# fp32 attention ahead of two MLPs: raw fp32 scores on row tiles, values held stationary on column tiles, GpSimd dividing the probabilities

## What is computed

```
scores = scale * q @ k^T                      # q and k are about 3 in size
scores = where(0 <= i - j < 128, scores + slope[head] * -(i - j), -1e9)
attn   = exp(scores - rowmax);  attn = attn / (rowsum + 1e-9)
x      = (attn @ v), heads side by side       # 2304 x 512
x      = gelu-like MLP (512 -> 2048 -> 512) of x
out    = a second MLP of the same sizes, with another activation
```

## Time and profile before

| what | value |
|---|---|
| median of 3 runs | 852.1 us |
| the profiled execution's own time | 850.05 us |
| its span, first to last instruction | 848.2 us |
| PE busy | 841.0 us (99%), 5744 matmuls |
| DVE, ACT, POOL busy | 711.7 us (84%), 538.4 us (63%), 116.5 us (14%) |
| granted TensorE clock | full in all 40 slices |
| attention | about the first 140 us |

### The profile page before, as it was taken

How to read it: one execution, slowest core, us unless ns; L and a number is a source line. 1 busy time by engine, 2 the same in 40 slices (tenths; PEclk the granted TensorE clock), 3 DMA queues, 4 the chain that set the end, 5 groups by cost and what they waited for, 6 DMA issues and landing times.

```text
span 848.2 us, 15510 instructions
## 1 busy us (share of the span) xinstructions
PE 841.0 (99%) x5744; PEld 836.5 (99%) x5744; DVE 711.7 (84%) x982; ACT 538.4 (63%) x791; POOL 116.5 (14%) x82
## 2 busy tenths in 40 slices
PE   8999999999999999999999999999999999999998
PEld 8999999999999999999999999999999999999998
DVE  7888898786988966778998897989989789889794
ACT  7778787676776546767744556767556566765441
POOL 3788988000000000000000000000000000000000
PEclk9999999999999999999999999999999999999999
DMA  8978671667776347686764862587646643888822
GB/s 199 227 207 227 186 187 68 257 256 283 241 256 223 135 163 273 241 303 246 261 241 185 298 227 122 199 282 267 233 162 247 231 153 141 296 290 295 304 106 75
DMA packets 63257, 186.45 MB, mean 220 GB/s; under 512 B 7504, under 2 KB 14352, under 8 KB 59344
## 3 DMA queue, kind: packets, MB, share of 16 engines
q1 hardware_dynamic: 62896, 185.30, 64.0%
q10 hardware_dynamic: 288, 0.16, 0.1%
HBM read 113.09 MB, written 72.35 MB: 219 GB/s over the span
## 4 chain that ended last, share of the span: by engine, by line
PE 91%; DVE 5%; POOL 1%; issue 1%; ACT 0%; DMA 0%; SPq 0%; DVEq 0%; POOLq 0%
PE ps L1075 79%; PE ps L1043 5%; PE ps L1009 3%; PE ps L1022 3%; DVE arena L1755 1%; POOL qk_hi L895 1%; PE ps L1037 1%; DVE probs L1645 1%; POOL k_lo L892 1%; PE ps L1052 1%; DVE qk_hi L1613 0%; DVE raw_first L1714 0%; DVE g L1787 0%; DMA qk_raw<-qkT 0%; DVE raw_first L1709 0%
## 5 line engine op out<-in xcount | busy, mean ns | idle before, releaser
L1075 PE MATMUL ps<-arena,w_first 128*128 128x384 f32 x1764 | 328.4, 336 | 0.0
L1075 PEld LDWEIGHTS ps<-arena,w_first 128*128 128x128 f32 x1764 | 307.3, 188 | 1.0 <-DVE arena L1755 0.6
L1075 PE MATMUL ps<-arena,w_rest 128*128 128x384 f32 x1260 | 240.0, 336 | 0.1
L1075 PEld LDWEIGHTS ps<-arena,w_rest 128*128 128x128 f32 x1260 | 220.1, 188 | 0.8 <-DVE arena L1755 0.4
L1755 DVE TENSOR_TENSOR arena<-raw_first,arena 128x768 fp32r<-128x768 f32 (+1 forms) x114 | 148.8, 1319 | 74.4 <-ACT arena L1333 74.1
L1333 ACT ACTIVATE arena<-raw_first 128x768 fp32r<-128x768 f32 (+1 forms) x120 | 132.0, 1117 | 46.1 <-DVE raw_first L1714 39.0
L1075 PE MATMUL ps<-w_rest,arena 128*128 128x256 f32 x945 | 130.8, 280 | 0.2 <-DVE g L1858 0.2
L1075 PEld LDWEIGHTS ps<-w_rest,arena 128*128 128x128 f32 x945 | 119.5, 189 | 0.4 <-issue 0.4
L1075 PE MATMUL ps<-w_first,arena 128*128 128x256 f32 x567 | 86.2, 279 | 0.0
L1755 DVE TENSOR_TENSOR arena<-raw_rest,arena 128x1536 fp32r<-128x1536 f32 (+1 forms) x48 | 71.3, 1486 | 7.1 <-ACT arena L1333 7.0
L1333 ACT ACTIVATE arena<-raw_rest 128x1536 fp32r<-128x1536 f32 (+1 forms) x48 | 60.9, 1269 | 22.4 <-PE ps L1075 20.2
(11 more groups left out here) (125 smaller groups left out, 971.0 us busy)
## 6 DMA issues: line engine op xcount, KB each, us to landing
gd<-g SPq DMA_DIRECT2D x24, 1536.0 KB, 6.1
raw_rest<-gd SPq DMA_DIRECT2D x32, 768.0 KB, 5.1
wst<-w_pairs SPq DMA_DIRECT2D x32, 512.0 KB, 5.7
raw_first<-gd SPq DMA_DIRECT2D x16, 768.0 KB, 6.0
yd<-ust SPq DMA_DIRECT2D x6, 1536.0 KB, 6.3
qk_raw<-qkT SPq DMA_DIRECT2D x30, 288.0 KB, 3.9
wd<-ust SPq DMA_DIRECT2D x4, 1536.0 KB, 8.8
raw_first<-yd SPq DMA_DIRECT2D x4, 1536.0 KB, 7.2
```

The costliest lines, as they stand in the source:

```text
L1075: last = nc.tensor.matmul(to, stationary, moving, start=start and n == 0, stop=n == len(steps) - 1, skip_group_check=True)
```

## The change

- Queries and keys are loaded once for both heads of a pair (head 0 on partitions 0 to 63, head 1 on 64 to 127), kept as plain fp32, and neither rounded nor split. Each score tile is one fp32 matmul over 64 rows; the two heads are issued alternately and lie on two row tiles of the array, each with its own PSUM bank.
- `accum_out` of the exponential gives the row sums. DVE adds 1e-9 and inverts them, once for items 0 to 3 and once for 4 to 8 of a pair, and POOL multiplies each of the nine items by its inverse, in place.
- PE transposes the divided probabilities (16 transposes a pair, in groups of four); ACT copies head 0's to `probs_t` and DVE head 1's.
- The values become the stationary operand (128x64) and the transposed probabilities the moving one (256, 128 or 64 columns), fp32, on two column tiles: head 0's output on partitions 0 to 63, head 1's on 64 to 127. The output is then already in the layout of `x_pairs`: the five last transposes go, and one DVE copy of 128x576 remains.
- The order goes by pairs. On PE: scores of pair q in two groups, transposes of q-1 (first group), values of q-2, transposes of q-1 (second group). `dve_gate` is now raised ahead of each of the nine items.
- At the seam the first two P1 products come ahead of the last transposes and values, then P6, P6, P5. The splits of S1 and S2 and the sums around them are placed anew among POOL, ACT and DVE; the split of S2 moves from POOL to DVE.

The core of the diff:

```diff
@@ PE: scores @@
-                for n_pass, k in enumerate((keys(qk_hi, head), k_lo[:, head % SPLIT_RING])):
-                    last = nc.tensor.matmul(place, queries, k[:, key0:key0 + BAND],
-                                            start=n_pass == 0 and (d > 0 or i == 0), stop=n_pass == 1 and (d > 0 or i == 1))
+        def wide_scores(q):
...
+                pe.wait_ge(scores_biased, made(q - 1, 3))
+            for blk in (2, 3):
+                for e in range(2):
+                    last = nc.tensor.matmul(score_bank[e][:, (blk - 2) * BAND:(blk - 1) * BAND], queries(q, e, blk),
+                                            keys(q, e, (blk - 1) * P, BAND), start=True, stop=True)
...
+        def other_scores(q):
...
+                pe.wait_ge(scores_biased, made(q - 1, 8))
+            for blk in (1, 0):
+                for e in range(2):
+                    place = score_bank[2 + e][:, 0:BAND] if blk else score_bank[2 + e][:, BAND:BAND + P]
+                    nc.tensor.matmul(place, queries(q, e, blk), keys(q, e, 0, BAND if blk else P), start=True, stop=True)
+            for part in range(2):
+                for e in range(2):
+                    last = nc.tensor.matmul(score_bank[2 + part][ROWS[e], 3 * P:3 * P + TAIL_HALF], queries(q, e, 4),
+                                            keys(q, e, SEQ - TAIL_KEYS + part * TAIL_HALF, TAIL_HALF), start=True, stop=True)
@@ PE: transposes and values @@
+        def transpose_wide(q):
+            for e in range(2):
+                pe.wait_ge(probs_scaled, made(q, 2 * e + 1))
+                wait_past(pe, pt_copied[e], 2 * q)
...
+        def transpose_others(q):
+            for e in range(2):
+                pe.wait_ge(probs_scaled, made(q, 6 + 2 * e))
+                pe.wait_ge(pt_copied[e], 2 * q + 1)
...
+        def weigh_values(q):
+            h = 2 * q % HEADS
+            for e in range(2):
+                pe.wait_ge(pt_copied[e], 2 * q + 2)
+            pe.wait_ge(v_in[q % BATCH_PAIRS], 32 * (q // BATCH_PAIRS + 1))
+            wait_past(pe, x_copied, q)
+            for blk in range(4):
+                width = BAND if blk < 3 else P
+                for e in range(2):
+                    nc.tensor.matmul(ps[ROWS[e], out_bank, blk * P:blk * P + width], v_sb[:, h + e, blk],
+                                     probs_t[:, q % 2, e, (2 * blk + 1) * P:(2 * blk + 1) * P + width],
+                                     start=blk == 0, stop=blk == 3, skip_group_check=True)
@@ PE: order @@
+        for q in range(PAIR_COUNT):
+            wide_scores(q)
+            other_scores(q)
...
+                transpose_wide(q - 1)
+                if q > 1:
+                    weigh_values(q - 2)
+                transpose_others(q - 1)
@@ POOL @@
-        def split_head(head):
...
+        def scale_probs(q, group):
+            pool.wait_ge(sums_inverted, 2 * q + group + 1)
+            for item in ((4, 5, 6, 7, 8) if group else (0, 1, 2, 3)):
+                at = prob(q, item)
+                nc.gpsimd.tensor_scalar(at, at, inverse[:, q % PROB_RING, item:item + 1], None,
+                                        ALU.mult).then_inc(probs_scaled, 1)
@@ ACT @@
+                nc.scalar.activation(at, at, ACT.Exp, bias=neg_max[:, q % PROB_RING, item:item + 1], scale=-1.0,
+                                     accum_out=inverse[:, q % PROB_RING, item:item + 1]).then_inc(probs_made, 1)
...
+        def copy_transposed(q, group):
+            act.wait_ge(probs_transposed, 4 * q + 2 * group + 1)
+            wait_past(act, pv_done, 2 * (q - 1))
@@ DVE @@
-            nc.vector.tensor_copy(loaded(qk_hi, head), loaded(qk_raw, head)).then_inc(qk_rounded, 1)
...
+        def invert_sums(q, group):
+            at = inverse[:, q % PROB_RING, 4:9] if group else inverse[:, q % PROB_RING, 0:4]
+            dve.wait_ge(probs_made, made(q, 8 if group else 3))
+            nc.vector.tensor_scalar(at, at, 1e-9, None, ALU.add).then_inc(sums_guarded, 1)
+            dve.wait_ge(sums_guarded, 2 * q + group + 1)
+            nc.vector.reciprocal(at, at).then_inc(sums_inverted, 1)
+        def copy_transposed(q, group):
+            dve.wait_ge(probs_transposed, 4 * q + 2 * group + 2)
+            wait_past(dve, pv_done, 2 * (q - 1))
...
+        for q in range(PAIR_COUNT):
+            bias_scores(q, (0, 1, 2, 3))
+            if q:
+                copy_transposed(q - 1, 0)
+            invert_sums(q, 0)
+            bias_scores(q, (4, 5, 6, 7, 8))
+            if q > 1:
+                copy_x(q - 2)
+            if q:
+                copy_transposed(q - 1, 1)
...
+            invert_sums(q, 1)
+        copy_transposed(PAIR_COUNT - 1, 0)
+        sum_operand(0, S2)
+        copy_x(PAIR_COUNT - 2)
+        split_half_weights(1)
+        copy_transposed(PAIR_COUNT - 1, 1)
...
+        split_operand(0, S2)
+        copy_x(PAIR_COUNT - 1)
```

More of the change, by code:

```diff
@@ L250, in wait_past @@
             engine.wait_ge(semaphore, count)
-    def pair_end(q):
-        return max(m for m, (pair, _) in enumerate(ORDER) if pair == q)
-    def pair_at(m, lag):
-        return next((q for q in range(PAIR_COUNT) if pair_end(q) + lag == m), None)
-    def group_of(m):
-        return next(i for i, (_, last) in enumerate(GROUPS) if last >= m)
-    def prob_place(m, i):
-        d = ORDER[m][1] - 1
-        return probs[:, d, i], 2 * d + i
-    def was_before(m):
-        q, d = ORDER[m]
-        return ORDER.index((q - 1, d)) if q else -1
@@ new lines, in keys, with queries, scores_of @@
+    def keys(q, e, first, count):
+        return qk[ROWS[e], q % QK_RING, KEYS_AT + first:KEYS_AT + first + count]
+    def queries(q, e, blk):
+        first = QUERIES_AT[blk]
+        return qk[ROWS[e], q % QK_RING, first:first + (P if blk < 4 else TAIL)]
+    def scores_of(item):
+        if item == TAIL_ITEM:
+            return ps[:, 2:4, 3 * P:3 * P + TAIL_HALF]
+        e, blk = ITEMS[item]
+        if blk >= 2:
+            return score_bank[e][:, (blk - 2) * BAND:(blk - 1) * BAND]
+        return score_bank[2 + e][:, 0:BAND] if blk else score_bank[2 + e][:, BAND:BAND + P]
@@ L1661, in copy_pair_tail, with bias_scores @@
-        def copy_pair_tail(q):
-            pair = q % BATCH_PAIRS
-            dve.wait_ge(pair_tail_transposed, q + 1)
-            for half in range(2):
-                rows = slice(half * TAIL, (half + 1) * TAIL)
-                last = nc.vector.tensor_copy(x_pairs[rows, pair, 4 * P:SEQ], xt_bank[rows, rows])
-            last.then_inc(pair_tail_copied, 1)
+        def bias_scores(q, items):
+            for item in items:
+                pair = q % BATCH_PAIRS
+                if q < BATCH_PAIRS:
+                    dve.wait_ge(bias_made, 3 * q + (3 if item == TAIL_ITEM else ITEMS[item][0] + 1))
+                dve.wait_ge(scores_ready, 4 * q + (4 if item >= TAIL_ITEM else 2))
+                wait_past(dve, probs_transposed, 4 * (q - PROB_RING) + (4 if item >= TAIL_ITEM else 2)
+                          if q >= PROB_RING else 0)
+                dve.sem_inc(dve_gate, 1)
+                if item == TAIL_ITEM:
+                    to, bias = (ap.rearrange("p (t n) -> p t n", t=2) for ap in (prob(q, item), bias_tail[:, pair]))
+                else:
+                    e, blk = ITEMS[item]
+                    to, bias = prob(q, item), bias_sb[:, 2 * pair + e, BAND - (P if blk == 0 else BAND):BAND]
+                nc.vector.tensor_tensor_reduce(out=to, in0=scores_of(item), in1=bias, scale=-SCALE, scalar=3.0e38,
+                                               op0=ALU.add, op1=ALU.min,
+                                               accum_out=neg_max[:, q % PROB_RING, item:item + 1]).then_inc(scores_biased, 1)
```

643 lines of the change are left out of this document (187 added, 456 removed).

## The result

The changed kernel takes 861.78 us (median, 861.09 to 863.15) against 851.85 for the kernel before: ratio 1.0118, 95% interval 1.0101 to 1.0136. It is slower by 9.9 us. The forecast was 834, faster; the range of 822 to 862 just holds the time, because it was drawn wide enough for the slower rivals; the forecast's own range ended at 843. The profiled execution took 861.25 us, with a span of 859.3.

A forecast was written before the change was run, and what follows sets the result against it. PE, busy 99%, was taken as the bound; pairs would fall from 8.06 to 7.0 us. Products would behave as if started at 117.6 + 3.5 + 1.8 + 2 x 0.9 = 124.7 us, not 143.1: 852.1 - 18.4 = 834 us, range 822 to 862.

The forecast's parts named there:

- slower rivals: Slower cases: fp32 tiles one after the other, 878 us (0.15); falling clock, 858 (0.08); POOL, 858 (0.07).
- POOL, the step that failed: POOL's nine one-input products a pair: 4.3 us, bounds 3.5 and 5.9, hidden under the 7.0 us pair.
- POOL is the bound: Rival: a per-partition factor costs more than a second input; at 1.0 us an item, 858 us; chance 0.07.
- Tiles in pairs: PE in attention: the two tiles run at once, taking PE's fp32 columns from 3.7 to 1.8 us a pair.
- At most 0.87 ns a column: PE's price for fp32 matmul columns, from the 130-column row: 3.7 us a pair before tile overlap.
- they overlap at 1.62 ns: Part of half a gain: tiles overlap on PE at 1.62 ns a column, giving a chain of 4.1 us.
- half a gain: Rival: PE's chain lengthens the pair to 7.6 us, 9.5 us back, 843 us; chance 0.25.
- The change of layouts: PE changes tile layout at least four times a pair, at 0.1 us each: 0.4 us a pair.
- The bias steps: DVE's nine bias items a pair, each with 0.035 us for the gate: 3.8 us, low 3.1.
- Start and seam: First product at 117.6 us; PE stands still 3.5 us at the seam; products behave as if started at 124.7.
- 4 us allowed for ACT: Half of ACT's some 8 us of bias tables and rounding, added to the 113.6 us before the first product.
- The clock rival: Rival: PE, mostly idle, drops to the low clock level; pair 8.5 us, 858 us; chance 0.08.

The follow-up runs named there:

- after: The changed kernel itself, as profiled, against the kernel before: 861.78 us, ratio 1.0118.
- e3: The changed kernel with POOL's division as a two-input multiply, the inverse broadcast as a second tensor of stride zero: 839.09 us.
- e2: The changed kernel with POOL multiplying by the constant 0.5 instead of the column of inverses, division left out: 847.92 us.
- e5: The changed kernel with DVE dividing the four 256-column items of a pair and POOL only the other five: 862.3 us.
- e4: The changed kernel without the division, and with score and value matmuls issued head by head, so neighbours use the same tile: 845.26 us.
- e1: The changed kernel without the division of the probabilities, PE's transposes waiting for the exponentials instead: 832.54 us, ratio to the kernel before 0.9786.

## Why the prediction was wrong

**POOL, the step that failed.** "I take 4.3, nearer the memset, as only one input is read": measured 7.3 us a pair. Even the upper bound, 5.9 from the two-input rows, was too low. "Even 5.9 is hidden under 7.0" fell with it: 7.3 us and the weight work of 0.7 to 1.3 us set the period of 8.21. The prediction assumed that one input costs no more than two, for which no row stood; 0.93 against 0.73 us in after, and 0.59 in e3, show that here it costs more. The rival "POOL is the bound" got 0.07 and is what happened: at 0.93 us an item its rule (7 us from 0.8, 8.5 at 1.0) gives about 8, and 8.21 was measured. It was named with the right place and sign, as a matter of the factor's price; e2 puts only 0.07 to 0.08 us on the factor. The Trainium skill (GPSIMD Engine Reference, Engine selection) calls one-input work roughly line rate and two-input work about twice slower than VectorE. The measurement decides: on POOL the one-input multiply was the slower of the two. Its advice to prefer VectorE for such work holds for the multiply alone, 0.26 us against 0.92, but beside POOL it gained nothing in e5.

**PE's columns.** Tiles in pairs: right (e4). The price: wrong by a factor of two. "At most 0.87 ns a column" came from 130-column starts; what was counted as one matmul was one of the two records that each fp32 matmul has in the traces. Alone, a 256-column matmul costs 1.68 ns a column, and 0.88 is the price with two tiles at work (0.84 without the change of layout ahead of them). The case "they overlap at 1.62 ns", which stood in half a gain, was the true one. PE has 6.1 us of work a pair in e1 and 0.2 of waiting, not 4.0 and 0.9. The change of layouts was under-priced too: 0.8 us a pair in e1, not 0.4. Transposes were right, 0.11 us each.

**DVE and ACT.** Copies of 512 and 576 columns cost 0.691 and 0.754 us, as forecast. The bias steps were overpriced: they follow each other every 0.345 us, so busy time over count, the low bound, was nearer than the mean of one with the gate's 0.035 on top. The gate cost nothing visible. DVE needs 5.7 us a pair in e1 (18.05 of 20 us), not 6.8. The sums' write-out costs ACT 0.09 us a step, as forecast: exponentials of 256 columns start 0.49 us apart, and 0.40 in the kernel before (a couple from 59.24 us took 0.90, one takes 0.50).

**Start and seam.** Forecast: first product 117.6 us, 7.1 more until the products behave as if started. Measured: 136.0 and 16.3. Of the 18.4 us to the first product, 14.8 are thirteen periods of 8.13 instead of 7.0 (20.33 to 126.08 us), 2.8 the start (pair 2 at 20.3, not 17.5), 4.8 the last pair, less the 4 us allowed for ACT. The start had missed that the first exponentials stand behind the tail's bias table, which landed late. The seam had PE waiting for S2 on DVE; in after it waited for POOL too, and the clock fell beside. In e3, with POOL out of the way, the first product comes at 117.35 us, but by other prices: shorter pairs and a longer start and last pair. The seam there is still about 5 us longer than forecast, which is the difference between 834 and 839.

**The clock rival** was right in direction and too large: the pairs did not stay at the low level. In after they had one short stretch of it, 0.66 from 105 to 110 us, in which a pair's wide values took 3.2 us instead of 1.7, and POOL went on at its pace: its pair there took 8.1 us (101.90 to 110.01). The windows at the start (0.83 from 10 to 20 us) and the seam (0.69 from 140 to 150 us) show the low level in part too, some 2 us in the products and values of the seam (2.26 against 1.20, 2.92 against 1.73).

**Left open:** why the one-input multiply is dearer on this engine than the two-input one (e3 changed the number of inputs and the operation together); whether the gaps on PE are the layouts'; and how much of the time around the seam is the clock, as no run here changed the clock alone.

## What to carry to other kernels

When work moves to an engine that was idle, its price there is the first thing to bound, and a bound from another operation, even one that reads more, is no bound: the same division cost 0.93 or 0.59 us by the choice of instruction, and the kernel was slower or faster than before by it. When work is moved between GpSimd and VectorE, ask what each does to the other: VectorE's four multiplies took 1.05 us beside an idle GpSimd and 1.9 beside a working one. Look at an engine's slices and windows, not at its share of the span: 17% was the bound of the first sixth. Where a trace has two records for one matmul, count the matmuls in the code before a duration becomes a price.

## What the runs showed of the hardware

- GpSimd, fp32 in place, 256 columns: one-input multiply by a column 0.92 us, by a constant 0.85, two-input with a stride-zero second input 0.59 to 0.62, with two full tensors 0.73. 128 columns: 0.60, 0.53 and, with a stride-zero second input, 0.40.
- POOL's multiply of 256 columns did not depend on DVE's work out of PSUM: from 136.9 to 138.8 us in after, where DVE mostly stood still, it took 922 ns, as in the busy pairs (924). Beside DVE's two-input operations it stretched: one of the two below took 1.71 us, the other 0.92. The groups of POOL in after, 140.7 to 146.3 us:

```profile
L783 POOL TENSOR_SCALAR probs<-probs,inverse 128x256 f32<-128x256 f32 x2 | 2.6, 1314 | 0.0
...
L783 POOL TENSOR_SCALAR probs<-probs,inverse 128x192 f32<-128x192 f32 x1 | 1.5, 1534 | 0.1
```

- A page on the last point: the Trainium skill (GPSIMD Engine Reference, Specifications) has the two engines share their access to SBUF, with contention when DVE reads two inputs from there; these rows agree (a mean of 1.31 against 0.92 us).
- It goes the other way too. DVE's one-input operations from SBUF to SBUF that started behind a two-input operation of GpSimd ended just behind it: in e5 twelve multiplies, 0.8 to 1.9 us instead of 0.35, each 0.15 us behind its end; in e3 the short addition of 1e-9, 0.17 us with GpSimd idle, took 0.29 to 1.44 beside GpSimd's weight work and ended 0.02 to 0.03 us behind it.
- Changes of layout on PE (128x128, two of 64x128, two of 64x64, two of 128x64): the starts around one lie 0.15 to 0.20 us further apart than within a layout, five times in a pair of e1.
- Of two tiles, matmuls of the second can start ahead of earlier ones of the first in the order: short head-by-head sequences of scores lost nothing, longer ones of values did.
- DVE's one-input multiply of 256 columns by a column of factors starts every 0.26 us with GpSimd idle, its biased copy out of PSUM every 0.345.
